# Low halves of w_in through TensorE, outputs read by ScalarE, new step tables and wide matmuls on zeros in a delta-rule and feed-forward kernel

## The reference, cut to what matters

```python
# attention: 4 batches x 8 heads, 768 tokens, head_dim 48
for t in range(S):
    y[:, :, t] = einsum('bhd,bhde->bhe', q[:, :, t], state)
    v_old = einsum('bhde,bhd->bhe', state, kt)                 # kt: normalised key
    state = state + bt * einsum('bhd,bhe->bhde', kt, vt - v_old)
x = y as (3072, 384)
h = maximum(x @ w_in, 0);  x = h * h @ w_out                    # w_in 384 x 2048
x = (sigmoid(x @ w_gate) * (x @ w_val)) @ w_last                # d_ff 1536
```

## Time and profile before

| what | value |
|---|---|
| median of 3 runs | 1092.68 us (1089.86 to 1094.75) |
| the profiled execution: its time, its span | 1100.69 us, 1098.9 us |
| PE busy | 1025.6 us (93%), DVE 563.3 (51%), ACT 440.9 (40%) |
| stage 0 | 0 to about 107 us |
| stage 1 (first with feed-forward blocks) | to about 223 us |
| stages 2, 3, 4, 5 | to about 321, 417, 515 and 607 us |
| stage 6, then the second layer | to 674 us, then to the end |

### The profile page before, as it was taken

The page is one execution under the profiler, slowest core; times in us unless marked ns, Lnnn a source line. Parts: engine busy times, 40 slices in busy tenths (PEclk is TensorE's granted clock), DMA queues, the critical chain, the costliest instruction groups (busy, mean ns, idle before and its releaser), DMA issues.

```text
span 1098.9 us, 24494 instructions
## 1 busy us (share of the span) xinstructions
PE 1025.6 (93%) x10653; PEld 555.6 (51%) x10653; DVE 563.3 (51%) x1088; ACT 440.9 (40%) x752; POOL 13.3 (1%) x27
## 2 busy tenths in 40 slices
PE   3398599989999999999999999999999999999997
PEld 2196256546646654764665444444444444444443
DVE  5956944983795487269614546143342343422422
ACT  4652154444445545444554784222222222222221
POOL 0000000000000000000000000000000000000000
PEclk7557699989999999999999999999999999999999
DMA  9505001500500230040300321001010010100000
GB/s 307 86 17 103 1 2 34 85 30 17 102 18 16 65 53 31 10 74 8 117 2 1 120 110 58 1 1 57 0 57 0 0 57 0 57 0 0 29 0 29
DMA packets 54856, 48.20 MB, mean 44 GB/s; under 512 B 45424, under 2 KB 49392, under 8 KB 54384
## 3 DMA queue, kind: packets, MB, share of 16 engines
q1 hardware_dynamic: 54336, 46.67, 16.5%
q10 hardware_dynamic: 432, 0.23, 0.1%
HBM read 37.45 MB, written 9.44 MB: 43 GB/s over the span
## 4 chain that ended last, share of the span: by engine, by line
PE 88%; DVE 9%; issue 2%; ACT 1%; DVEq 0%; POOL 0%; POOLq 0%
PE psum L550 69%; PE psum L488 3%; PE psum L501 3%; PE psum L476 2%; PE psum L427 2%; PE psum L424 2%; PE psum L461 2%; DVE attn L897 2%; DVE attn L895 2%; DVE work L956 1%; PE psum L450 1%; PE psum L514 1%; PE psum L438 1%; DVE work L954 1%; ACT attn L631 1%
## 5 line engine op out<-in xcount | busy, mean ns | idle before, releaser
L550 PE MATMUL psum<-work,attn 128*128 128x512 f16 x1944 | 419.9, 379 | 0.1
L550 PE MATMUL psum<-work,w 128*128 128x512 f16 x1728 | 392.5, 385 | 18.0 <-DVE work L937 16.7
L550 PEld LDWEIGHTS psum<-work,attn 128*128 128x128 f16 x1944 | 190.1, 98 | 229.8 <-DVE work L956 0.6
L550 PEld LDWEIGHTS psum<-work,w 128*128 128x128 f16 x1728 | 166.5, 99 | 220.5 <-issue 18.3
L631 ACT ACTIVATE work<-work 128x512 f16<-128x512 f32 (+1 forms) x264 | 155.8, 624 | 156.0 <-DVE work L1111 139.9
L1111 DVE SCALAR_TENSOR_TENSOR work<-psum,work 128x512 f32<-128x512 f32 x72 | 49.8, 692 | 269.8 <-PE psum L550 258.8
L631 ACT ACTIVATE attn<-psum 32x512 f32<-32x512 f32 (+4 forms) x168 | 81.5, 500 | 130.6 <-PE psum L476 39.2
L631 ACT ACTIVATE work<-psum 128x512 f32<-128x512 f32 x96 | 57.1, 595 | 138.8 <-PE psum L550 138.3
L631 ACT ACTIVATE work<-psum,scal 128x512 f32<-128x512 f32 x72 | 49.4, 686 | 138.5 <-PE psum L550 137.8
L937 DVE SCALAR_TENSOR_TENSOR work<-work 128x512 f16<-128x512 f16 x96 | 66.2, 689 | 71.0 <-ACT work L631 69.2
L897 DVE TENSOR_TENSOR attn<-attn 128x31 f32<-128x31 f32 (+15 forms) x186 | 63.7, 343 | 6.4
(11 more groups left out here) (79 smaller groups left out, 585.1 us busy)
## 6 DMA issues: line engine op xcount, KB each, us to landing
attn<-in_kt SPq DMA_DIRECT2D x24, 192.0 KB, 4.1
attn<-in_v SPq DMA_DIRECT2D x6, 768.0 KB, 5.7
attn<-in_kn SPq DMA_DIRECT2D x6, 768.0 KB, 7.1
x_spill<-work SPq DMA_DIRECT2D x6, 768.0 KB, 3.3
xt<-x_spill SPq DMA_DIRECT2D x6, 768.0 KB, 4.9
y_out<-work SPq DMA_DIRECT2D x6, 768.0 KB, 3.6
attn<-in_qt SPq DMA_DIRECT2D x20, 192.0 KB, 4.7
work<-in_w_out SPq DMA_DIRECT2D x1, 3072.0 KB, 21.8
```

The costliest lines, as they stand in the source:

```text
L550: m = mm(dst, x, z, start=first and i == 0, stop=last and i == len(a) - 1)
```

## The change

1. **Low half of w_in.** The VectorE pieces (`first_weights_in`) go. TensorE makes the difference in PSUM, 12 pieces of 128x512: an fp32 matmul of the identity times the scale with the raw weights, and an fp16 matmul of minus the identity with the high half; ScalarE copies each to fp16 (`rest_of_first`, `cut_rest_first`). Ten pieces stand in step OPEN, two at step 10 of stage 0. They use banks 2, 3, 4 and 1.
2. **Output.** `read_out` moves from VectorE to ScalarE.
3. **Tables.** PLACE, OTHER, STEP_US, FIRST_US and SCALE_COLUMNS have new numbers, which move fills and VectorE jobs in every stage.
4. **Matmuls on zeros.** The 14 near the end of the columns go; 20 stand between pieces 8 and 9 of item 1; two stand ahead of each mid, off, qk, ks and dr fill of stage 0 (15 fills).

```diff
-PLACE = dict(rows=2, scale_v=7, mid=(6, 6), off=(6, 7), qk=(2, 4, 7, 9), ks=(7, 16), dr=(12, 16), ...
+PLACE = dict(rows=4, scale_v=8, mid=(8, 8), off=(10, 10), qk=(-4, 4, 8, 12), ks=(10, 14), dr=(12, 15), ...
...
-STEP_US = 1.5
-FIRST_US = 1.75
+STEP_US = 1.3
+FIRST_US = 0.75
...
-SCALE_COLUMNS = (18, 28)
-WARM_START, WARM_MID, WARM_END = 11, 14, 12
+SCALE_COLUMNS = (10, 24)
+REST_BANKS, REST_PIECES = 4, 12
+REST_FIRST = (4, 6)
+WARM_START, WARM_MID, WARM_END = 11, 20, 12
+WARM_AHEAD = ("mid", "off", "qk", "ks", "dr")
...
-                    if s == 0 and step != OPEN:
-                        if kind == "mid" and x == 0:
-                            pe.wait_ge(lane_step, L_ROWS - 10)
-                            keep_clock(WARM_MID)
+                    if s == 0 and step > OPEN and kind in WARM_AHEAD:
+                        keep_clock(2)
...
+            def rest_of_first(n):
+
+                if n >= REST_BANKS:
+                    pe.wait_ge(w_lo_done, n - REST_BANKS + 1)
+                if n == 0:
+                    pe.wait_ge(w_hi_done, 1)
+                    pe.wait_ge(idents_ready, 2)
+                at = slice(TOK * n, TOK * (n + 1))
+                to = rest_bank[n % REST_BANKS]
+                mm(to, scaled_ident, raw_a[:, at], start=True, stop=False)
+                mm(to, minus_ident, w1h[:, 0:part][:, at], start=False, stop=True).then_inc(rest_full, 1)
...
+                    if s == 0 and step == OPEN:
+                        for n in range(sum(REST_FIRST)):
+                            if n == 2 * REST_BANKS:
+                                keep_clock(WARM_MID)
+                            rest_of_first(n)
...
+            def read_out(m):
+                act.wait_ge(slot_free, N1 * (m + 1) + SLOTS)
+                act.wait_ge(x2_stored, 16 * (m + 1))
+                act.wait_ge(f_step, 2 * m + 2)
+                for j in range(KC):
+                    run(outst[:, j], o_bank[j], scale=cell((OUT_B, OUT_C)[m % 2])).then_inc(o_read, 1)
...
+            def cut_rest_first(n):
+
+                act.wait_ge(rest_full, n + 1)
+                run(w1h[:, part + TOK * n:part + TOK * (n + 1)], rest_bank[n % REST_BANKS]).then_inc(w_lo_done, 1)
...
-            def first_weights_in(kc):
-
-                at = slice(FF1 * kc, FF1 * (kc + 1))
-                if kc == 0:
-                    dve.wait_ge(w_hi_done, 1)
-                V.scalar_tensor_tensor(out=w1h[:, part:2 * part][:, at], in0=raw_a[:, at], scalar=cell(WI + 2),
-                                       in1=w1h[:, 0:part][:, at], op0=ALU.mult, op1=ALU.subtract).then_inc(w_lo_done, 1)
```

More of the change, by code:

```diff
@@ L124, in other_work @@
         us += 0.7
-    if step == 0 and s > 1:
-        us += 2.4
     return us
@@ L180, in delta_rule_ffn_kernel @@
         v_bank = [psum[:, b, :] for b in (5, 6)]
+        rest_bank = [psum[:, b, :] for b in (2, 3, 4, 1)]
         sizes = dict(kt=2 * UN * CH, pq=UN * 2 * CH, kn=UN * CH, v=UN * HD, gp=UN * CH, e=UN * CH, dr=UN * BL,
@@ L240, in delta_rule_ffn_kernel @@
         outst = work[:, o:o + KC * TOK].rearrange("p (k t) -> p k t", k=KC)
+        o = KC * FF1
+        scaled_ident = work[:, o:o + P]
+        minus_ident = work[:, o + P:o + P + P // 2].bitcast(F16)
         mask_s = sb("mask_s", 2 * CH)
@@ L586, in stage @@
                     attention(s, step)
+                    if s == 0 and step == OPEN:
[3 more added lines that the diff above has]
+                            rest_of_first(n)
+                    for n in range(sum(REST_FIRST), REST_PIECES):
+                        if s == 0 and step == place(0, "rest")[n - sum(REST_FIRST)]:
+                            rest_of_first(n)
             pe.wait_ge(zeroed, 1)
@@ L716, in cut_first, with scale_ident @@
                 run(hi, raw, scale=cell(at_cell + 2)).then_inc(w_hi_done, 1)
+            def scale_ident():
+                act.wait_ge(w_step, W_STEPS)
+                run(scaled_ident, ident_s[:], scale=cell(WI + 2)).then_inc(idents_ready, 1)
+            def cut_rest_first(n):
+                act.wait_ge(rest_full, n + 1)
+                run(w1h[:, part + TOK * n:part + TOK * (n + 1)], rest_bank[n % REST_BANKS]).then_inc(w_lo_done, 1)
             def cut_small(n):
@@ L756, in stage @@
                         hidden_square_lo(k, s - 1)
+                    if s > 1 and step == 0:
+                        read_out(s - 2)
                     if 0 < s < GROUPS and step == place(s, "rows") + 1:
@@ L762, in stage @@
                         root_k(0)
+                        act.wait_ge(in_const, 48)
+                        run(minus_ident, ident_s[:], scale=-1.0).then_inc(idents_ready, 1)
                         weight_squares(raw_a[:], WI, w1[:, 0:part], "wi", 32)
+                        weight_root(0, WI)
+                        scale_ident()
+                        cut_first(0, raw_a[:], WI, w1h[:, 0:part])
                         weight_squares(raw_o, WO, w1[:, part:2 * part], "wo", 16)
-                        weight_root(0, WI)
-                        cut_first(0, raw_a[:], WI, w1h[:, 0:part])
                         weight_root(1, WO)
+                        for n in range(REST_FIRST[0]):
+                            cut_rest_first(n)
                         cut_first(1, raw_o, WO, w1h[:, 2 * part:3 * part])
+                        for n in range(REST_FIRST[0], sum(REST_FIRST)):
+                            cut_rest_first(n)
                         place_e(0)
@@ L787, in _ @@
                 stage(s)
+            read_out(GROUPS - 1)
             with act.Fori(0, GROUPS) as g:
@@ L1003, in first_weights_out @@
                                        in1=w1h[:, 2 * part:3 * part][:, at], op0=ALU.mult, op1=ALU.subtract)\
[L1004 removed]
+                    .then_inc(w_out_done, 1)
             def second_weights(k):
@@ L1025, in stage @@
                     k, odd = divmod(step, 2)
-                    if s > 1 and step == 0:
-                        read_out(s - 2)
                     if s > 0 and not odd and 1 <= k <= N1:
@@ L1048, in stage @@
                         evacuate(*f)
-                    for n in range(KC):
-                        if s == 0 and step == place(0, "first_in")[n]:
-                            first_weights_in(n)
                     if chain and step == place(s, "xmax"):
@@ L1081, in stage @@
                         split_x(x2_split, GROUPS)
-                if not chain:
-                    read_out(GROUPS - 1)
             dve.sem_inc(glo_ready, 2)
```

24 lines of the change are left out of this document (10 added, 14 removed).

## The result

| | before | after |
|---|---|---|
| median of the runs compared | 1093.7 us (4 runs, 1089.9 to 1101.5) | 1078.1 us (4 runs, 1077.6 to 1079.4) |
| ratio, 95% interval | | 0.984 (0.980 to 0.988) |
| profiled execution, its span | 1100.7, 1098.9 | 1078.2, 1076.3 |

The change makes the kernel 1.6% faster, 15.6 us between these medians. Three later comparisons timed the kernel before in 23, 8 and 23 further runs, with medians of 1095.9, 1096.3 and 1096.9. So some 18 us is the better figure, although the kernel after was timed in these four runs only. The forecast was 1070.5 us with a range of 1062 to 1086.

What follows compares the result with a forecast made beforehand. TensorE was taken to bound: a fixed sum of work from the first feed-forward block, plus waits and lower clock. Gains of 9.6 + 9.6 + 3.0 = 22.2 us off 1092.7 gave 1070.5 us, range 1062 to 1086.

Steps and rivals of the forecast that it cites:

- start of h0: First feed-forward block of stage 1 on TensorE: starts at 97.2 us instead of 106.8, a gain of 9.6 us.
- losses in stage 1: TensorE time lost to waits and lower clock in stage 1: falls from 26.1 to 16.5 us, a gain of 9.6.
- stages 2 to 5: Waits at stage ends (2.9 us) and of off for mid (1.4) go, p1 waits 1.3 more: gain 3.0 us.
- that gap is hidden: End of stage 0: with the split ahead of to_lanes, the 4.2 us issue gap in the last kk no longer delays.
- The wait for p0: Stage 1: after h0, h1, h2 and a qk end at 104.3, TensorE waits 11.6 us for VectorE's L0 at 115.8.
- The piece of the low half: Step OPEN on TensorE: one fp32 matmul of 128x512 takes 1.03 us, 1.25 with its fp16 partner, at full clock.
- Moving read_out costs nothing: Stage ends: ScalarE's three reads, some 1.8 us, fit before its next job; VectorE saves 2.25 us a stage without bounding.
- Dropping the pieces from VectorE gains nothing by itself: Stage 0: VectorE's three w_in pieces, some 7 us, lay beside TensorE's work, so removing them alone wins no time.
- The clock of stage 0: TensorE's granted clock, 0.50 from 51 to 91 us before, taken to hold near 1.0 from 54 to 89 us.
- my first rival: Stage 0: clock falls after mid until kk, 27 us later, 1097; chance 0.07, 0.20 for up to half the chain.
- The third rival: Stages 1 to 5: the tables don't do what they say, VectorE holds L1 or the split; 1083 us, chance 0.10.
- I find no reason for the losses to be only the profiled run's: Whole kernel: the 22.2 us saved in the profiled execution of 1100.7 also come off the median, 8.0 us lower.

Runs made afterwards that it cites:

- a_late_load: Kernel after, with SyncE issuing the next group's kn and q loads behind the last kk fill of stage 0: 1077.2 us, ratio 0.985 to the kernel before.
- a_low_dve: Kernel after, with w_in's low halves made by VectorE again and 20 zeros in place of the ten pieces: 1074.2 us, ratio 0.980 to the kernel before.
- b_pairs: Kernel before, plus only two zero matmuls ahead of each mid, off, qk, ks and dr fill of group 0: 1095.9 us, ratio 1.000.
- a_no_pairs: Kernel after, without the pairs of zero matmuls ahead of group 0's fills: 1080.2 us, ratio 0.985 to the kernel before.
- a_old_place: Kernel after, with the old table of steps and STEP_US for stages 1 to 5: 1087.4 us, ratio 0.992 to the kernel before.
- b_again: Kernel before, unchanged, run again: 1097.7 us, ratio 1.002, its profiled execution 1097.85.
- b_late_load: Kernel before, with SyncE waiting for the last kk fill of group 1 before it loads kn and q: 1093.3 us, ratio 0.998.

## Why the prediction was right or wrong

**The direction and the profiled execution.** The sum said 22.2 us less for the profiled execution, and the spans differ by 22.6. That they lie so close is in good part luck, since the parts were not what I had put down:

| term | forecast | measured |
|---|---|---|
| start of h0 | 9.6 | 2.0 (106.80 to 104.80) |
| losses in stage 1 | 26.1 to 16.5: 9.6 | 26.1 to 10.2: 15.9 |
| stages 2 to 5 | 3.0 | 4.7 (the rest of 22.6) |

For stage 1 I subtract as the prediction did: the same work took 124.5 us before (106.80 to 231.29), and 108.6 after (104.80 to the qk at 216.41, less the block and the qk that now stand ahead of it, 3.05). What the trace shows of the loss that is left is 6.76 + 1.38 + 0.72 of waits and 1.95 of cold matmuls in p0 (3.97 less 2.02), 10.8 in all; the 0.6 between the two is within the rounding of the prices (a block took 1.96 us, not 2.0). The 4.7 hold some 1.8 us of lower clock in stage 4 of before (0.91 over 420 to 440 us), which the prediction had left out as chance.

**The step that failed first: "that gap is hidden".** The gap moved with the kk fill, stayed 4.64 us long and lay ahead of h0 on TensorE itself. Behind it the clock was down: the rest of the fill took 1.25 us more than in a_late_load (2.78 against 1.53), the two zeros 0.4, qk 0.8. With 0.2 from the end of xt and 0.2 of waiting ahead of the fill that is 7.5 of the 7.6 us between 104.8 and 97.2. I had asked only whether the split would wait for the gap, not whether TensorE would. a_late_load shows it: h0 at 99.94.

**Why it cost so little.** h0's start and the wait for p0 are no independent terms. VectorE sets p0: its first column came 2.8 us later than forecast (107.6), L993 at 117.9 + 0.7. The wait for p0, forecast 11.6, was shortened by 7.6 on one side and lengthened by 2.8 on the other, to 6.8. The forecast for p0 was wrong by 2.8 us only. So 4.8 of the 7.6 us missing at h0 came back in the row of stage 1 because the two are coupled, and that isn't luck; the rest of the close fit is.

**Sizes in stages 1 and 2.** Off behind mid 1.4: measured 1.38. The 0.9 of clock there was not lost. Cold start of p0 2.6: 1.95. End of stage 1, 0: right. p1 of stage 2, 1.3: 0.80. Issue gaps of 3.6 us in all behind 118 us I had not counted.

**The piece of the low half.** I took 1.25 us with its partner; it measured 1.08 (0.86 + 0.22, row at 42.66). This is where the Trainium skill (FP8 and Floating Point Precision, TensorE Precision Notes) said four passes for true fp32: by that rule 1.1, and the trace agrees. The nearest row, a transpose, was the poorer guide, by 1.4 us over eight pieces; the late start at the lower level and mid's read at 57.4 (forecast 58.2) came out within a microsecond.

**"Moving read_out costs nothing; it saves VectorE 2.25 us a stage, where VectorE no longer bounds"**: half wrong. It cost nothing, and it gained 6.4 us. My sum had priced the removal at zero, as VectorE, busy for 64 of 96 us in stage 3, "no longer bounds". But the reads stand ahead of the columns and of L1, and in stage 2 TensorE waits for that stretch, 3.0 us more with the reads in it; the other 3.4 us of the 6.4 no wait explains. My own forecast of a wait for L1 in stage 2 named the place where those 2.25 us count.

**"Dropping the pieces from VectorE gains nothing by itself"**: right, and the other side of it, 3.5 us later off and 2.5 in the chain, was in the sum; a_low_dve gets 4.05 of it back at p0.

**The clock of stage 0.** It held, as taken (1.00 from 54 to 84 us). But that was not the term it seemed. b_pairs has it from 66 us on and gains nothing; a_no_pairs loses it for a few us (my first rival, in part) and is within 2 us. The third rival, tables that don't do what they say, fell: a_old_place puts the table of stages 1 to 5 at 9.3 us, against the 3.0 I had given stages 2 to 5, though how much of the 9.3 is chance clock isn't shown. (The 1083 of that rival doesn't come out of its own terms: 8.2 for the stages, 1.4 and the 6.8 at the end of stage 1 on top of 1070.5 make 1087.)

**The median.** 1070.5 against 1078.1: the step that failed is "I find no reason for the losses to be only the profiled run's". The profiled execution of before stood 8.0 above a median of three. b_again puts its profiled execution at the median, and 54 later runs put the median near 1096: about 4.7 of the 8 us were that one execution, with its low clock of 0.947, and 3.3 a low median of three. The kernel after has no such distance (1078.17 against 1078.14). Set against 1096, the sum would have given 1074; without the 4.7 us of losses that were that execution's alone, 1078.5. So the sum held for the one execution that it was read from, and the step from it to the median did not.

## What to carry to other kernels

A start time and the wait behind it must be priced as one thing: find the engine that sets the far end of the wait, and take only how much earlier that engine gets there. An engine's free share of a stage says nothing of the piece of work that stands ahead of its dense stretch; putting a job of 2 us a stage back there cost 6.4 us, where the old table cost 9.3. And one profiled execution beside three runs is too little to carry microseconds from one to the other where the clock of each run differs: ask how the clock of the profiled one compares.

## What the runs showed of the hardware

TensorE can stand still inside a fill, with no semaphore to wait for, while other queues move many small packets: 3.5 to 4.9 us in ten traces, in nine of them ending 8.1 to 10.4 us after the issue of a load of 768 KB (kn). Moving the load away left gaps of 1.2 to 2.4 us, so part of it needs no such packets: the gap of 2.42 us in b_late_load has 37 packets beside it over 86 to 90 us. Whether TensorE waited for its instructions the traces don't say, though the packets of the instruction queue fit it (above).

Issue gaps of 0.2 to 1.6 us stand at the same places of the program in several kernels (a kk fill at 338 to 352 and another at 432 to 446 us), with different lengths. Two gaps of 0.66 us at the same instruction were followed by matmuls at the lower level in one trace and at the higher in the other (above), 1.7 us apart. A few such places would make the several microseconds between runs of one kernel; that they do isn't shown, since only profiled runs have traces.

The clock came back by itself in stage 0 of the kernel without pairs, in b_late_load (0.57 over 50 to 70 us, 0.98 over 70 to 90), and also in b_again, where it read 0.57 and 0.66, against the 0.50 of the earlier trace rows for the same program. What tells these apart, the runs don't show.
